# Unit 1's loads placed behind the maximum and the first rows, other counts of products of ones, and a new order of work in groups 32 to 36 of a fused mLSTM, MoE and gated MLP kernel

## What is computed

```python
m_new = maximum(f_gate[t] + m, i_gate[t])
C = exp(f_gate[t] + m - m_new) * C + exp(i_gate[t] - m_new) * outer(v[t], k[t])
n = exp(f_gate[t] + m - m_new) * n + exp(i_gate[t] - m_new) * k[t]
y[t] = sigmoid(o_gate[t]) * (C @ q[t]) / maximum(abs(n @ q[t]), 1)
...
x = sum over e of p[:, e] * (relu(y @ w1[e]) @ w2[e])      # 4 experts of 1024
out = ((x @ w_a) * (x @ w_b)) @ w_out                       # 1536 wide
```

## Time and profile before

| | us |
|---|---|
| median of 3 runs | 614.17 (613.86 to 615.46) |
| the profiled execution, its own time | 615.42 |
| its span | 613.2 |
| PE busy (of the span) | 602.8 (98%) |
| DVE busy | 357.8 (58%) |
| ACT busy | 291.3 (47%) |
| POOL busy | 179.3 (29%) |

### The profile page before, as it was taken

The page is one execution under the profiler, slowest core; times in us unless marked ns, Lnnn a source line. Parts: engine busy times, 40 slices in busy tenths (PEclk is TensorE's granted clock), DMA queues, the critical chain, the costliest instruction groups (busy, mean ns, idle before and its releaser), DMA issues. The chain is left out here.

```text
span 613.2 us, 10973 instructions
## 1 busy us (share of the span) xinstructions
PE 602.8 (98%) x4009; PEld 582.9 (95%) x4009; DVE 357.8 (58%) x705; ACT 291.3 (47%) x618; POOL 179.3 (29%) x246
## 2 busy tenths in 40 slices
PE   7999999999999999999999999999999999999997
PEld 6888999999999999999999999998789999999996
DVE  6577974554473444543536444497786665666555
ACT  3888744424443444443444434655644443444332
POOL 4456430014340134301334001515024530453000
PEclk8999999999999999999999999999999999999999
DMA  4665531002311021410022100221101410120011
GB/s 127 206 212 178 169 125 41 20 1 68 96 39 61 1 46 32 125 40 23 20 49 86 57 12 0 47 58 55 51 12 39 116 56 12 38 54 1 1 66 64
DMA packets 21092, 38.39 MB, mean 63 GB/s; under 512 B 3552, under 2 KB 11344, under 8 KB 21040
## 3 DMA queue, kind: packets, MB, share of 16 engines
q1 hardware_dynamic: 19040, 35.02, 20.1%
q10 hardware_dynamic: 2000, 2.69, 1.3%
HBM read 26.42 MB, written 1.97 MB: 46 GB/s over the span
## 5 line engine op out<-in xcount | busy, mean ns | idle before, releaser
L1629 PE MATMUL PS<-w2h,hh 128*128 128x320 f32 x528 | 164.9, 312 | 1.7 <-DVE acc L1230 0.9
L1629 PE MATMUL PS<-w2l,hh 128*128 128x320 f32 x528 | 163.7, 310 | 0.0
L1629 PE MATMUL PS<-w2h,hl 128*128 128x320 f32 x528 | 163.1, 309 | 0.0
L1548 PE MATMUL PS<-xop,wop 128*128 128x384 f32 x400 | 139.0, 348 | 1.6 <-DVE c_s L1208 0.6
L1551 PE MATMUL PS<-xop,wop 96*128 96x384 f32 x400 | 135.1, 338 | 0.0
L1549 PE MATMUL PS<-xop,wop 128*128 128x384 f32 x400 | 134.8, 337 | 0.0
L1550 PE MATMUL PS<-xop,wop 128*128 128x384 f32 x400 | 134.7, 337 | 0.0
L721 ACT ACTIVATE hh<-c_s 128x384 fp32r<-128x384 f32 x120 | 62.8, 524 | 101.9 <-DVE c_s L1208 28.7
L1629 PEld LDWEIGHTS PS<-w2h,hh 128*128 128x128 f32 x528 | 99.5, 188 | 3.1 <-DVE hl L1185 3.0
L1629 PEld LDWEIGHTS PS<-w2l,hh 128*128 128x128 f32 x528 | 99.6, 189 | 0.0
L1629 PEld LDWEIGHTS PS<-w2h,hl 128*128 128x128 f32 x528 | 99.4, 188 | 0.0
(11 more groups left out here) (148 smaller groups left out, 816.2 us busy)
## 6 DMA issues: line engine op xcount, KB each, us to landing
s<-in_wt SPq DMA_DIRECT2D x24, 256.0 KB, 3.2
kvo<-in_tok SPq DMA_DIRECT2D x12, 480.0 KB, 4.4
wop<-t1h SPq DMA_DIRECT2D x48, 112.0 KB, 2.2
qk<-in_qk_t SPq DMA_DIRECT2D x24, 160.0 KB
s<-in_w SPq DMA_DIRECT2D x12, 320.0 KB, 3.0
wop<-t1l SPq DMA_DIRECT2D x24, 112.0 KB, 2.2
s<-in_w_out SPq DMA_DIRECT2D x12, 160.0 KB, 2.2
out_y<-acc SPq DMA_DIRECT2D x12, 160.0 KB, 1.9
```

What stands on the lines that cost most here:

```text
L1548: nc.tensor.matmul(to, ws[0], xs[0], start=opens, stop=False, skip_group_check=True)
L1629: got = nc.tensor.matmul(bank, left, (w2l if part == 1 else w2h)[p][:, f, :], start=opens and part == 0, stop=closes and part == 2)
```

## The change

Five edits, none of which adds or removes arithmetic.

1. SP issues unit 1's `qk` loads behind the copy of the maximum and both first high rows, and no longer ahead of them; `load_dec_l(1)` moves from ACT's queue to SP's, ahead of `load_rows(2)`.
2. `keep_busy(5)` becomes 9 (ahead of `log_weights(0)`), `keep_busy(4)` becomes 1 (ahead of `products(1)`).
3. `chunks` for groups 33 and 34.
4. ACT in the gated groups: `keep_u2` and the second `keep_turn` go ahead of `prepare_early`; `x_high` 4 goes behind `keep_u2`.
5. DVE in the gated groups: group 33 adds three tiles ahead of `make_c11`; `x_sum` 1, `x_low` 4 and `x_low` 5 of a set move later by some steps, and `low_w2(19)` from group 35 to group 36.

```diff
@@ chunks @@
-                return (3, 6, 1, 0, 6, 6, 1, 6, 4, 3) if n <= FIRST else (0, 5, 1, 0, 4, 4, 0, 3, 1, 0)
+                return (3, 6, 1, 0, 6, 6, 1, 6, 4, 3) if n <= FIRST else (0, 5, 0, 0, 4, 5, 0, 4, 0, 0)
@@ SP @@
             load_kvo(0)
-            sp.wait_ge(qk_zero, 2)
-            load_qk(1)
             sp.wait_ge(m_ready, 1)
             sp.dma_start(m_r[:, 1, :], m[:, P + 1:S + 1]).then_inc(m_in, 16)
             load_first_high_row(0)
             load_first_high_row(1)
+            sp.wait_ge(qk_zero, 2)
+            load_qk(1)
             load_kvo(1)
+            load_dec_l(1)
             load_rows(2)
@@ ACT @@
-            load_first_dec_l()
...
                 replicate_late(b2, 5)
-                if b3 is not None:
-                    x_high(b3, 4)
                 if n > FIRST:
                     high_product(n - 1, 1)
                 if b4 == 2:
                     x_high(b4, 6)
+                keep_u2(n)
+                if b3 is not None:
+                    x_high(b3, 4)
+                keep_turn(n, 1)
                 prepare_early(n)
-                keep_u2(n)
-                keep_turn(n, 1)
                 keep_turn(n, 2)
@@ DVE, gated_group @@
+                if n == FIRST + 1:
+                    add_tiles(n, range(HB, UB))
                 make_c11(n)
+                if b3 is not None:
+                    x_sum(b3, 1)
+                if b4 is not None:
+                    x_low(b4, 5)
                 if n > FIRST:
                     low_product(n - 1, 1, c12_s[:, :])
-                if p == 1:
+                if p == 1 and n > FIRST + 1:
                     add_tiles(n, range(HB, UB))
-                if n > FIRST:
+                if b1 is not None:
                     w2_lows(n - 1)
-                if b1 is not None:
                     x_low(b1, 0)
                 if b2 is not None:
+                    w2_lows(n - 1)
                     x_sum(b2, 0)
                     x_low(b2, 2)
...
-                if b4 == 2:
-                    x_low(b4, 5)
                 if b4 is not None:
                     x_low(b4, 6)
+                if n == FIRST + 4:
+                    w2_lows(n - 2)
+                if n > FIRST + 3:
+                    w2_lows(n - 1)
                 make_c22(n)
...
+                make_c12(n)
+                low_product(n, 0, c11_s[:, :])
                 if b3 is not None:
                     x_low(b3, 4)
-                make_c12(n)
-                if b2 is not None:
-                    x_sum(b2, 1)
-                low_product(n, 0, c11_s[:, :])
                 make_ab2(n)
                 if b1 is not None:
                     x_low(b1, 1)
-                if b3 is not None:
-                    x_low(b3, 5)
@@ PE @@
             products(0)
-            keep_busy(5)
+            keep_busy(9)
             log_weights(0)
             turn_first_logs()
             log_weights(1)
-            keep_busy(4)
+            keep_busy(1)
```

More of the change, by code:

```diff
@@ L637, in late_high @@
                     nc.scalar.activation(xop[1][:, 0:2, at], raw_q(3), ACT.Copy).then_inc(late_hi, 1)
[L639 to L644, removed]
             def load_first_low_row(b):
```

## The result

The changed kernel takes **618.24 us** (median of nine executions, 617.91 to 622.08), the kernel before took 614.71 us beside it (median of nine). The ratio is 1.0064, 95% interval 1.0044 to 1.0085: slower by 3.9 us (2.7 to 5.2), beyond the 0.3% that can be told apart. The forecast was 615.0 us, with a range up to 617.4: it was wrong, too low.

A forecast was written before the change was run, and what follows sets the result against it. PE, busy 602.8 of 613.2 us, was taken as the bound. Terms -2.3 - 1.6 + 4.05 - 0.48 + 1.2 = +0.9 us gave 616.3 us for the profiled execution, 615.0 against the median; range 612.5 to 617.4.

The forecast's parts named there:

- From the execution to the median: Whole kernel: the profiled execution's 1.25 us over the median was taken off, from 616.3 to 615.0 us.
- The clock: Behind group 36's stop: the clock falls to 1.2 GHz, partly within the stop; +1.2 us, bounds 0 and 1.7.
- The start: Kernel start: earlier maximum, fewer products of ones and a held clock bring `products(1)` forward; -2.3 us, bounds -2.6 and -0.9.
- 13.1 us is the latest: Kernel start: unit 1's `qk`, issued at about 9.4 us and taking 3.7 us, is there by 13.1 us.
- if the attention shows waits of PE for `dec_l`: Attention, in the profile after: such waits would mean that the gain at the start was lent; no size given.
- Groups 33 to 35: Second layer there: PE's stops for a late `acc` and two low parts `hl` go; -1.6 us, bounds -2.2 and -1.1.
- POOL's moved splits: Groups 33 to 35: they might meet `x_low` 0 and `x_sum` 0 on DVE, taking back at most 1.0 us.
- Group 36: Second layer of group 35 waits there for `low_w2(19)`; PE comes to it 4.05 us later, bounds 3.6 and 4.4.
- PE stands for nearly 5 us: In group 36: PE is ready some 2.4 us after P6 of group 35, then waits for `low_w2(19)`.
- The chain of DVE's rows: From P6 of group 35 to the matmul needing `low_w2(19)`: DVE's queued steps take 7.24 us, before 3.19.
- the return: From the delayed matmul to P0 of group 37: 6.75 us becomes 6.27 with inputs ready, -0.48 us.
- The slower rival: Start gives only half (-1.1) and the clock falls, costing its full 1.7: sum +2.6, 616.8 us; chance 0.25.

The follow-up runs named there:

- fed_stop: The changed kernel with 20 unread identity products in PE's queue just ahead of group 36's second layer; 616.27 us, ratio 1.0034 to the kernel before.
- after_again: The changed kernel run once more, unaltered, beside the kernel before; 619.06 us, ratio 1.0047.
- late_alone: The kernel before with only `low_w2(19)` moved from group 35 to group 36, ahead of `make_c22`; 619.75 us, ratio 1.0067.
- mid_only: The kernel before with the reordering of groups 33 to 36, `low_w2(19)` left in group 35, start unchanged; 611.88 us, ratio 0.993.
- w2_back: The changed kernel with `low_w2(19)` put back in group 35, ahead of `x_low` 3; 612.65 us, ratio 0.997 to the kernel before.
- mid_mr: mid_only with 9 and 1 products of ones and the maximum's copy ahead of unit 1's `qk`; 611.53 us, ratio 0.9939 to the kernel before.
- w2_soon: The changed kernel with `low_w2(19)` directly behind `make_c11` of group 36; 614.37 us, ratio 0.9984 to the kernel before.
- sp_alone: The kernel before with only the start's edits of SP's and ACT's queues; 614.41 us, ratio 0.9982.
- mid_busy: mid_only with 9 and 1 products of ones in place of 5 and 4; 611.50 us, ratio 0.994 to the kernel before.
- qk_mid: w2_back with unit 1's `qk` directly behind the maximum, ahead of the first rows; 611.77 us, ratio 0.9925 to the kernel before.

## Why the forecast was wrong

The forecast stood at 616.3 us for a profiled execution; after's was 618.21. The forecast for the median was 615.0; measured were 618.24. So 1.9 us are the sum's, and 1.3 us the step from the execution to the median. Of the 1.9, the clock makes +1.5 and the start +0.9, groups 33 to 36 -0.1, and -0.3 lie outside all terms.

- **The clock, "+1.2 us (bounds 0 and 1.7)": this is the term that failed most.** That the clock falls was right, and the stop on `w2l` is its cause (fed_stop). Its cost is 2.6 to 2.7 us. I took it from the one place with a low clock in the trace of before, where 1.7 us were lost between 12 and 16 us. That row bounds nothing: the clock was at half for 3.4 us there, and for 6.8 us behind this stop. That part of the fall would lie in the stop, where it is free, was right (1.2 us of the 6.8), but I took it off a price that had no such part in it. Two stops of 4.83 and 3.68 us cost the same 2.7 us of slow work behind them; one of 2.02 us cost none. The rule quoted there from the Trainium skill ("TensorE: Matmul & The Clock Gate", section "Why this matters for your kernels": long idle gaps put the clock back to half) agrees, fed_stop being the direct test; that section gives no price.
- **The start, -2.3 us (bounds -2.6, -0.9): -1.41, inside the bounds.** The maximum came as early as forecast (8.81 us), and the clock held. What failed is "13.1 us is the latest" for unit 1's `qk` (it was used at 14.02): I took the 3.7 us of `kvo` from the first issue, but the two `qk` transfers take 1.13 us to issue, and the second was there 4.6 us after the first was begun. `qk` bounds the step now, and p, there at 13.22 us, would have bounded it next. The sign "if the attention shows waits of PE for `dec_l`" doesn't stand in after's profile, but it does in after_again's: 0.8 us at 25.3 us, and P0 of group 33 at 420.75, 0.7 us behind the 420.07 of an undisturbed start of before.
- **From the execution to the median, -1.25 us: counted twice.** The profiled execution of before lay 1.25 us over the median of three executions (0.7 over that of the nine), and its clock fell at the start. Of the 99 executions of before beside the experiments, 53 kept a mean clock of 0.999 or 1.000. The start's gain contained the end of that fall. The changed kernel's profiled execution, 618.21, lay on its median. What is taken out by the change can't be taken off once more to get to the median. Against late_alone's execution, whose clock held, the start wins 0.5 us.
- **Groups 33 to 35, -1.6 us: -1.84.** All three stops went. POOL's moved splits did meet `x_low` 0 and `x_sum` 0, as the forecast weighed, but each took only 0.4 us longer (0.93 for 0.55, and 1.32 for 0.95), and PE waited for neither.
- **Group 36, 3.6 to 4.4 us, "PE stands for nearly 5 us": +4.19 and 4.83 us.** The chain of DVE's rows (7.24 against 7.38 us) and the return (-0.48) were right; late_alone shows the step acting alone.
- **The slower rival** (the start gives half and the clock falls, 616.8 us) was nearest to what happened. Its sum of +2.6 means 618.0 us for the profiled execution, where 618.21 were measured, but that is partly luck: its clock was 1.0 us too cheap, and its other terms together 0.8 us too dear. What it fell short by in the median is nearly all the 1.25.

## What to carry to other kernels

A helper step that a later tensor-engine step needs must be queued by its use and not by where there is room: walk the queue of the engine that makes it, from the last thing that releases that queue, and compare with when it is wanted. A stop of TensorE can cost more than its length: in these groups, stops of 3.7 and 4.8 us brought 2.7 us of slow work behind them and one of 2.0 us nothing, while in the start and the attention stops of 1.1 to 2.7 us stood ahead of slow stretches (next section). So its length alone gives no price; before accepting such a stop, shorten it or fill it (mid_only has no such stop, and is 0.7% faster where the whole change is 0.6% slower). And when the time of a profiled execution is over the median, look for what made it so before pricing an edit against it.

## What the runs showed that I had not expected

The length of a slow stretch isn't fixed. At the stops in group 36 it is 6.8 us in both kernels (the clock is 0.53 over 453 to 460 us, 0.51 over 455 to 462). In the attention it can be far longer. w2_back, profiled execution, a wait of PE and three stretches:

```profile
25.55 0.38 PE L1432 MATMUL PS<-mask,identb 128*128 128x512 bf16 x1 [1.41 <-DMA dec_l<-alo_r]
```

```profile
16.00:26.00 10.00, 8.29 (x93) 6.60 (x92) 6.11 (x18) 6.99 (x18) 3.65 (x5) 1.00 0.67 189
26.00:39.50 13.50, 13.50 (x83) 11.21 (x82) 4.03 (x11) 6.67 (x16) 3.99 (x5) 0.50 0.52 173
39.50:75.00 35.50, 35.50 (x395) 30.40 (x392) 26.58 (x65) 28.14 (x68) 21.78 (x26) 1.00 0.55 178
```

One small copy that landed 1.4 us late, with the DMA engines at 0.67, was followed by 13.5 us at half rate with PE busy all the time, about 6.8 us lost: this execution took 618.85 us, the lowest of the same kernel 610.73. The other profiled executions say the same: behind a stop of 1.24 us came 3.4 us at half rate (before), behind 1.63 also 3.4 (mid_only), behind 1.65 it was 6.8 (mid_mr), behind 1.20 it was 24 (w2_soon), behind 1.12 it was 44 (sp_alone) and behind 2.71 it was 65 us (mid_busy). Behind 1.39 us in the start of qk_mid and 1.20 in that of w2_soon came none. So the length of a stop predicts neither whether the clock falls nor for how long. Why the copy lands late in some executions only, and what sets the length of the slow stretch, is open. No run here varied either by itself.
